# An mLSTM layer with two gated layers on one core: decay products first in each group, the causal mask as a select on GpSimd, loops written out

## The reference

```python
for t in range(S):
    m_new = np.maximum(f_gate[:, :, t] + m, i_gate[:, :, t])
    f_stab = np.exp(f_gate[:, :, t] + m - m_new)
    i_stab = np.exp(i_gate[:, :, t] - m_new)
    m = m_new
    C = f_stab * C + i_stab * np.einsum('bhd,bhe->bhde', vt, kt)
    n = f_stab * n + i_stab * kt
    h_tilde = np.einsum('bhde,bhe->bhd', C, qt)
    denom = np.maximum(np.abs(np.einsum('bhd,bhd->bh', n, qt)), 1.0)
    y[:, :, t] = sigmoid(o_gate[:, :, t]) * h_tilde / denom
x = y as (1536, 320)
xn = x / rms(x) * rms_g
x = (silu(xn @ w_gate) * (xn @ w_val)) @ w_out                 # 320 -> 1536 -> 320
h = x @ w_in; g = max(h, 0) + alpha * min(h, 0)                # 320 -> 2048
out = g @ w_out2                                               # -> 320
```

## Time and profile before

| | |
|---|---|
| median of 3 runs | 508.81 us (507.23 to 510.04) |
| profiled execution | 508.86 us, of which 507.1 us are the span from the first to the last instruction |
| mean granted TensorE clock | 0.996 |
| TensorE busy | 484.6 us (96%) |
| VectorE busy | 319.0 us (63%) |
| GpSimd busy | 233.8 us (46%) |
| ScalarE busy | 212.7 us (42%) |

### The profile page before, as it was taken

How to read it: one execution, slowest core, us unless ns; L and a number is a source line. 1 busy time by engine, 2 the same in 40 slices (tenths; PEclk the granted TensorE clock), 3 DMA queues, 4 the chain that set the end, 5 groups by cost and what they waited for, 6 DMA issues and landing times.

```text
span 507.1 us, 9931 instructions
## 1 busy us (share of the span) xinstructions
PE 484.6 (96%) x3161; PEld 464.2 (92%) x3161; DVE 319.0 (63%) x647; ACT 212.7 (42%) x508; POOL 233.8 (46%) x250
## 2 busy tenths in 40 slices
PE   5998899999999999999999799999999999998996
PEld 4887889998999999998999799999899999997996
DVE  7585896757796484547887366437769622236663
ACT  1442436256535324236545222234654432235652
POOL 3540767536657134244657124331756622225673
PEclk9999999999999999999999899999999999999999
DMA  6778431123434670003435490002243420004562
GB/s 109 165 139 168 129 95 58 51 68 88 114 92 111 121 105 0 1 1 84 124 85 135 90 145 2 1 0 54 88 115 88 89 65 2 1 0 115 137 123 99
DMA packets 80735, 41.31 MB, mean 81 GB/s; under 512 B 51548, under 2 KB 80684, under 8 KB 80684
## 3 DMA queue, kind: packets, MB, share of 16 engines
q1 hardware_dynamic: 80684, 40.65, 35.3%
HBM read 38.67 MB, written 1.97 MB: 80 GB/s over the span
## 4 chain that ended last, share of the span: by engine, by line
PE 75%; DVE 9%; issue 8%; POOL 3%; ACT 2%; DMA 1%; ACTq 0%; DVEq 0%; POOLq 0%; SPq 0%
PE bank L984 36%; PE bank L992 17%; PE bank L995 8%; PE bank L948 2%; PE bank L936 2%; PE bank L912 1%; POOL w L845 1%; DMA shared<-in_moe_w_out 1%; PE bank L889 1%; PE bank L943 1%; POOL hidT L853 1%; PE bank L954 1%; PE bank L926 1%; PE bank L884 1%; PE bank L927 1%
## 5 line engine op out<-in xcount | busy, mean ns | idle before, releaser
L853 POOL TENSOR_TENSOR hidT<-hid,hidT 128x384 fp32r<-128x384 f32 x112 | 118.2, 1055 | 232.3 <-ACT hidT L513 232.0
L513 ACT CAST hidT<-hid 128x384 fp32r<-128x384 f32 x112 | 57.5, 514 | 135.7 <-DVE hid L741 94.1
L984 PE MATMUL bank<-x2T,win 128*128 128x384 f32 x512 | 100.2, 339 | 1.4 <-ACT x2T L554 0.8
L984 PEld LDWEIGHTS bank<-x2T,win 128*128 128x128 f32 x512 | 87.5, 188 | 3.2 <-issue 1.7
L735 DVE SCALAR_TENSOR_TENSOR u<-th,bank 128x384 f32<-128x384 f32 x48 | 26.6, 554 | 92.0 <-ACT th L535 92.0
L984 PE MATMUL bank<-xT,wg 128*128 128x384 f32 x384 | 75.7, 339 | 4.6 <-issue 2.8
L984 PE MATMUL bank<-xT,wv 128*128 128x384 f32 x384 | 77.3, 344 | 0.0
L984 PEld LDWEIGHTS bank<-xT,wg 128*128 128x128 f32 x384 | 66.3, 189 | 6.2 <-issue 5.1
L992 PE MATMUL bank<-w,hidT 128*128 128x320 f32 x384 | 68.4, 313 | 3.5 <-POOL w L845 3.5
L984 PEld LDWEIGHTS bank<-xT,wv 128*128 128x128 f32 x384 | 67.5, 191 | 1.2 <-DVE hid L741 0.3
L758 DVE TENSOR_SCALAR u<-bank,alpha_sb 128x384 f32<-128x384 f32 x64 | 39.4, 616 | 42.3 <-PE bank L984 41.6
(11 more groups left out here) (129 smaller groups left out, 638.2 us busy)
## 6 DMA issues: line engine op xcount, KB each, us to landing
shared<-in_moe_w_out SPq DMA_DIRECT2D x38, 320.0 KB, 5.1
shared<-in_moe_w_in SPq DMA_DIRECT2D x34, 256.0 KB
shared<-in_moe_w_in SPq DMA_DIRECT2D x34, 128.0 KB
q_in<-in_q SPq DMA_DIRECT2D x12, 160.0 KB, 4.4
k_in<-in_k SPq DMA_DIRECT2D x12, 160.0 KB, 4.6
v_in<-in_v SPq DMA_DIRECT2D x12, 160.0 KB, 4.3
o_in<-in_o_gate SPq DMA_DIRECT2D x12, 160.0 KB, 4.4
shared<-in_moe_w_gate SPq DMA_DIRECT2D x6, 256.0 KB
```

Of the source, the lines that this page charges most:

```text
L513: a.copy(hidT[:, i % NH, 0], hid[:, i % 2]).then_inc(s_hid_hi, 1)
L853: gp.tensor_tensor(hidT[:, i % NH, 1], hid[:, i % 2], hidT[:, i % NH, 0].bitcast(F32), ALU.subtract).then_inc(s_hid_lo, 1)
L984: last = te.matmul(dst, w[:, blk, col:col + P], x[:, part, xb, :], start=(n == 0), stop=(n == len(terms) - 1))
```

## The change

These things are changed together.
- In each group D0 and D1 stand ahead of the q and k transposes. So the k transposes now wait for D1's exponential (both use A[2]), D1 waits for `gt_tok` or for C instead (they read A[2]), and `gx` is computed behind D1's exponential. The `norm` of the group before stands between `kT` and S as before, GpSimd's `decay_rhs` for the next group is built at S and `state` instead of D1 and S.
- The mask product is gone. In its place GpSimd zeroes the upper part of `dx` by a select (`causal`), one for each half of the heads, and VectorE's pT waits for it.
- `upd` and `pairmask` are gone; two adds, one for each half of the partitions, take the diagonal blocks from the bank into C.
- The loops over tiles, and SyncE's over weight blocks, are Python loops.
- `maskF` and `maskR` go; the fillers multiply by the identity.

```diff
-    ATT += [("qT", _g), ("kT", _g)] + [("norm", _g - 1)] * (_g > 0) + [("D0", _g), ("D1", _g), ("S", _g)]
+    ATT += [("D0", _g), ("D1", _g), ("qT", _g), ("kT", _g)] + [("norm", _g - 1)] * (_g > 0) + [("S", _g)]
...
-            with eng.Fori(1, NT - 1) as t:
+            for t in range(1, NT - 1):
                 walk(MERGED, mlp, att, weights, t, t + 1)
...
-                with sp.Fori(0, J2 // 4 - 1) as m:
+                for m in range(J2 // 4 - 1):
...
-            with sp.Fori(1, NT - 1) as t:
+            for t in range(1, NT - 1):
...
@@ ScalarE
                     a.copy(kT[0:KP, :, :], quad(A[2])[0:KP]).then_inc(s_kT, 1)
-                    if g == 0:
-                        act.wait_ge(s_gexp_in, t + 1)
-                        act.wait_ge(s_kw, BACK + G * t)
-                        a.activation(gx[:, :, :, :], gexp_in[:, :, :, :], ACT.Exp).then_inc(s_gx, 1)
...
                     a.activation(dx[:, half], quad(A[2 * half]), ACT.Exp).then_inc(s_dx, 1)
+                    if g == 0 and half:
+                        act.wait_ge(s_gexp_in, t + 1)
+                        act.wait_ge(s_kw, BACK + G * t)
+                        a.activation(gx[:, :, :, :], gexp_in[:, :, :, :], ACT.Exp).then_inc(s_gx, 1)
@@ VectorE
-            for r, one in ((0, 0), (REM, 1)):
-                vec.memset(pairmask[r:r + REM, one], 1.0).then_inc(s_const_dve, 1)
-                vec.memset(pairmask[r:r + REM, 1 - one], 0.0).then_inc(s_const_dve, 1)
...
-            vec.tensor_copy(maskR[:, :], maskF[:, :]).then_inc(s_const_dve, 1)
...
                         dve.wait_ge(s_S_mm, BACK + 2 * n + half + 1)
-                        dve.wait_ge(s_dx, 2 * n + half + 1)
+                        dve.wait_ge(s_causal, 2 * n + half + 1)
...
-                    dve.wait_ge(s_upd, n + 1)
+                    dve.wait_ge(s_state_mm, BACK + n + 1)
                     dve.wait_ge(s_C_dec, n + 1)
-                    vec.tensor_tensor(C[0:KP], C[0:KP], upd[0:KP], ALU.add).then_inc(s_C, 1)
+                    for half in range(2):
+                        own = slice(HP * half, HP * half + D)
+                        last = vec.tensor_tensor(C[own, half::2], C[own, half::2], heads(A[2])[own, half::2], ALU.add)
+                    last.then_inc(s_C, 1)
...
-                elif what == "state":
-                    dve.wait_ge(s_state_mm, BACK + n + 1)
-                    dve.wait_ge(s_C, BACK + n)
-                    vec.tensor_tensor(upd[0:KP, :, :].rearrange("p (a b) d -> p a (b d)", b=2), heads(A[2])[0:KP].rearrange("p (a b) d -> p a (b d)", b=2),
-                                      mid(pairmask[0:KP, :, :].rearrange("p b d -> p (b d)"), KP, PAIRS, 2 * DA), ALU.mult).then_inc(s_upd, 1)
@@ GpSimd
-            gp.affine_select(out=maskF[:, :], in_=maskF[:, :], compare_op=ALU.is_ge, fill=-BIG, base=0,
-                             pattern=[[1, P]], channel_multiplier=-1).then_inc(s_const, 1)
...
+            def causal(n, half):
+
+                pool.wait_ge(s_dx, 2 * n + half + 1)
+                gp.affine_select(out=dx[:, half], in_=dx[:, half], compare_op=ALU.is_ge, fill=0.0, base=0,
+                                 pattern=[[0, H // 2], [1, CH]], channel_multiplier=-1).then_inc(s_causal, 1)
...
-                elif what in ("D1", "S") and g < G - 1:
-                    decay(n + 1, g + 1, int(what == "S"))
+                elif what in ("D0", "D1"):
+                    causal(n, int(what[1]))
+                elif what in ("S", "state") and g < G - 1:
+                    decay(n + 1, g + 1, int(what == "state"))
@@ TensorE
-                        pe.wait_ge(s_gate_step, GATE_STEPS * (t + 1)) if g == 0 else pe.wait_ge(s_upd, n)
+                        pe.wait_ge(s_dx, 2 * n + 2)
...
                     if half:
-                        pe.wait_ge(s_kT, n + 1)
+                        pe.wait_ge(s_C, BACK + n) if g else pe.wait_ge(s_gate_step, GATE_STEPS * (t + 1))
...
-                    te.matmul(quad(A[2 * half]), decay_lhs[0:KQ, g * CH:(g + 1) * CH], decay_rhs[0:KQ, half::2, :], start=True, stop=False)
-                    te.matmul(quad(A[2 * half]), identR[:, :], mid(maskR[:, :], P, H // 2, CH), start=False, stop=True).then_inc(s_D_mm, 1)
+                    te.matmul(quad(A[2 * half]), decay_lhs[0:KQ, g * CH:(g + 1) * CH], decay_rhs[0:KQ, half::2, :], start=True, stop=True).then_inc(s_D_mm, 1)
```

More of the change, by code:

```diff
@@ L173, in program @@
         hsum = sb("hsum", [P, H, DA])
-        upd = sb("upd", [P, H, DA])
-        pairmask = sb("pairmask", [P, 2, DA])
         den = sb("den", [P, 3, H])
@@ L202, in program @@
         identR = sb("identR", [P, P], F32R)
-        maskF = sb("maskF", [P, P])
-        maskR = sb("maskR", [P, P], F32R)
         sel = sb("sel", [P, H])
@@ L265, in program @@
         s_dx = sem("s_dx")
+        s_causal = sem("s_causal")
         s_S_mm = sem("s_S_mm")
@@ L272, in program @@
         s_state_mm = sem("s_state_mm")
-        s_upd = sem("s_upd")
         s_C_dec = sem("s_C_dec")
@@ L315, in program @@
         s_group = [sem(f"s_group{g}") for g in range(G)]
-        N_CONST, N_CONST_DVE, GATE_STEPS = 14, 16, 3 * G + 6
+        N_CONST, N_CONST_DVE, GATE_STEPS = 12, 11, 3 * G + 6
         BACK = 3
@@ L800, in _ @@
                 pool.sem_inc(held, BACK)
-            for ap, value in ((ident[:, :], 0.0), (maskF[:, :], 0.0), (sel[:, :], 0.0), (minus_half[:, :], -0.5),
+            for ap, value in ((ident[:, :], 0.0), (sel[:, :], 0.0), (minus_half[:, :], -0.5),
                               (q_in[:, :, :, D:HP], 0.0), (k_in[:, :, :, D:HP], 0.0), (kw[:, :, D:HP], 0.0), (v_in[:, :, :, D:DA], 1.0)):
                 gp.memset(ap, value).then_inc(s_const, 1)
-            pool.wait_ge(s_const, 8)
+            pool.wait_ge(s_const, 7)
             gp.affine_select(out=ident[:, :], in_=ident[:, :], compare_op=ALU.not_equal, fill=1.0, base=0,
                              pattern=[[-1, P]], channel_multiplier=1).then_inc(s_const, 1)
-            gp.affine_select(out=maskF[:, :], in_=maskF[:, :], compare_op=ALU.is_ge, fill=-BIG, base=0,
-                             pattern=[[1, P]], channel_multiplier=-1).then_inc(s_const, 1)
             for r in range(4):
-                pool.wait_ge(s_const, 10 + r)
+                pool.wait_ge(s_const, 8 + r)
                 gp.affine_select(out=sel[:, :], in_=sel[:, :], compare_op=ALU.not_equal, fill=1.0, base=-32 * r,
@@ L883, in _ @@
             for _ in range(WARM_UP):
-                te.matmul(quad(GV[1]), identR[:, :], mid(maskR[:, :], P, 4, CH), start=True, stop=True)
+                te.matmul(quad(GV[1]), identR[:, :], mid(identR[:, :], P, 4, CH), start=True, stop=True)
             def keep(count):
                 for _ in range(count):
-                    te.matmul(quad(GV[1]), identR[:, :], mid(maskR[:, :], P, 4, CH), start=True, stop=True)
+                    te.matmul(quad(GV[1]), identR[:, :], mid(identR[:, :], P, 4, CH), start=True, stop=True)
             def att(what, g, t):
@@ L964, in att @@
                     elif g == 1:
-                        pe.wait_ge(s_upd, G * t + G)
+                        pe.wait_ge(s_C, BACK + G * t + G)
                     else:
```

## The result

The kernel became slower: 515.49 us, median of 4 runs (515.1 to 515.68), against 508.68 us for the kernel before on the same chip (4 runs, 507.23 to 510.04). The ratio is 1.0135, 95% interval 1.0108 to 1.0161. The forecast was 508.1, slightly faster, with a range of 503.8 to 512.0; the kernel is 6.8 us slower and lies above that range. The profiled execution took 515.31 us with a span of 513.5, that is 6.4 us of span more than before.

The account below looks back on a forecast made before the run. TensorE, busy 96% of the span, was taken to bound the kernel. From 508.86 us: -2.8 and +0.6 (mask product), -4.5 (loops), +2.8 (opening), +2.9 (first tile), +0.2 (looped tiles) gave 508.1, range 503.8 to 512.0.

Parts of the forecast that it names:

- step 3: Opening, 11 to 46 us: D0 and D1 first lengthen the serial chain; +2.8 us, bounds +1 and +4.
- Rival G: Opening: the clock falls there too, as TensorE idles 1.3 and 0.6 us; +1.7 us, 509.8; chance 0.06.
- Step 2: Loops written out: the stall at the jump back and the slow clock behind it go; together -4.5 us.
- Rival F: Jump between tiles: the stop at 284 us stays in straight code; 4.5 us more, 512.6; chance 0.08.
- Step 1: Mask product removed on TensorE: -2.8 us in the two looped tiles, +0.6 given back at the `out2` 0 wait.
- step 5: Looped tiles: D0 stalls 0.1 us each for its right-hand side, other new waits are covered; +0.2 us.
- Step 4: First tile: D0 waits 4.2 us for GpSimd's `decay_rhs` and the clock falls behind it; +2.9 us.
- rival C: First tile: TensorE waits, but the clock stays up; 1.7 us less, 506.4; chance 0.13.
- B: First tile: TensorE does not wait, as GpSimd reaches the decays earlier; 4.3 us less, 503.8; chance 0.11.
- D: Opening costs only 0.5 us, as fillers give way and exponentials overlap the transposes; 505.8; chance 0.12.
- rival E: GpSimd's select costs much more than its rows scale to, deciding from about 1.2 us on; +5 us, 513; chance 0.08.

## Why the prediction was wrong

**What failed is step 3, the opening**: +8.8 where it had +2.8, outside its own bounds of +1 and +4. Two things in it were off, and only the second is large.

The chain itself, at full clock, came to +4.2 instead of +2.8 (the kernel with fillers). Group 0 was right: S +1.6 at 17.14, the walk said 17.1. From there to S of group 1 it grew by 0.85 (walk 0.6), from `hsum` to S of group 2 by 1.7 (walk 1.5). The rest is in the parts on VectorE. The walk took 0.9 off between S of group 1 and its `hsum`, because `upd` goes; measured is -0.3. There the scaling of C, 0.92 before, takes 1.32. It now begins near the start of a weight split on GpSimd, where before it began near its end, and so most of the saved 0.49 is given back. Between S of group 2 and its `hsum` it grew by 0.4 where the walk had nothing.

The clock cost 4.6 us. The step put D0 at 13.4 and wrote "Before, the transposes of q and k lay in the time of that wait", and didn't ask what TensorE does in that time once they are gone: it idles for 2.47 us, and again for 0.68 and 1.49 before the later groups. Rival G named the effect, but at 1.3 and 0.6 us of idleness, one fall of the clock and 1.7 us, with a chance of 0.06. The prediction itself had, for the first tile, the premise that an idle stretch brings the clock down; it was not applied to the one place of the kernel where TensorE has the least to do. The opening is a serial chain with nothing to hide a slow stretch behind, and here there were several in a row.

**Step 2, the loops, was right**: -4.5 forecast, -4.4 measured with this edit alone. Rival F is out.

**Step 1, the mask products, was right in size and nearly in sum.** In the old order a tile gains 1.40, so the 0.2 a tile that I set against `out2` 0 did not show there; with D0 first 0.38 a tile comes back, against 0.3 forecast (0.2 in step 1, 0.1 in step 5).

**Step 5 failed at "Other new waits are covered"**: 0.84 a tile in three tiles, by the decay product that moved to `state`. I checked the queue of each engine for what stands behind what, but not what runs beside what. The kernel with both decays at S shows it: that one step moved takes the wait away.

**Step 4, the first tile: the sum hit (+2.6 against +2.9, and 0.2 from step 1), the wait was right, and the clock term was wrong.** D0 starts 4.06 us later than the q transposes stood, forecast 4.2. Only 2.33 of it is idleness, because TensorE's clock fell behind the stall of 1.78 us for `u` and it came to D0 late; but GpSimd's right-hand side sets D0's start, so this low clock cost nothing more. Behind the wait for D0, where I had put 1.7 for the clock, it stayed full, as rival C had it. Two terms that I didn't have took its place: 0.59 for the low clock that the opening left behind in the first `gate` projections, and 0.84 for the x2 transposes. With what goes (six masks 1.4, the waits of 0.6 for `gt_tok` and 0.5 for the exponential) this gives 4.06 + 0.59 + 0.84 - 2.5 = +3.0, against 2.63 measured; some 0.3 is not accounted for. That the sum agreed is luck: 1.7 that did not come stood for 1.4 that were left out. Taking D0's wait away gave back 1.94 and no more, since the low clock behind the stall then counts. B (no wait) and D (a cheap opening) are out.

**The select.** 0.61 forecast, 0.64 measured without other work beside it (median; the mean in the changed kernel is 0.72): rival E is out. The sentence "At either it is hidden" was wrong as a general claim. In the old order the opening is 2 us longer with the select. It queues behind `norm`, and pT waits 1.3 us for it; moving `norm` gave back 0.57. Doubling it makes the opening up to 2 us longer again, part of that by the clock. In the changed order `norm` stands behind the selects, and no wait for pT stands in the list of TensorE's waits. The two adds to C were put at 0.32 each and took 0.323.

What stays open: why the 1.78 us stall in the first tile brings the clock down in some kernels and not in others (below). In the changed kernel it costs nothing, as it lies in the wait for D0; in the three kernels without that wait (weight pieces behind the gates, and the two with repairs) D0 starts 9.36 or 9.37 us behind the stall, against 7.81 for the step at that place before. Some 0.3 us of the first tile stay open too.

## What to carry to other kernels

An order that puts a step first puts it ahead of its input as well: for each such step look up what the engine did in the time of the wait, and in a serial stretch put work or fillers there, or the clock is lost on top of the wait (here 4.6 us on 4.2). But ask of a slow stretch what it delays: where the next step waits for another engine anyway, it costs nothing. When a step moves, look at what it will run beside, not only at what is queued behind it: VectorE and GpSimd products in the same stretch took 1.3 to 2.7 times as long as with nothing beside them. And take bundled changes apart: here loops, select and state gained 5.0 us in the old order (503.3 against 508.3), and the reordering that came with them cost 12.2 (515.5 against 503.3).

## What the runs showed of the hardware that was not expected

- The clock does not follow the length of a single stall. Every one of these kernels has the same wait of 1.78 us for `u` in the first tile. From 1 us before its end to 7 us behind, the granted clock was 0.79 in nine of them (the changed kernel, its four single repairs, the two with repairs together, all but the order, each select twice) and 1.00 in five (the kernel before, only the loops, loops and select, all but the order with more fillers, the same with `norm` moved). Before the last `xT` transposes of the opening, 2.34 and 2.35 us of idleness left the clock at 1.00 (old order in the opening only, repairs together), while 2.34 and 2.33 us were followed by 0.50 for at least 2 us (loops and select, 48 to 50 us; all but the order, 46 to 48 us).
- A product on GpSimd beside VectorE's slows both: 1.04 to 1.36 us on GpSimd, 1.31 to 2.16 for two splits on VectorE. The scaling of C takes 0.49 with nothing beside it and 1.32 in group 1 of the changed opening, beside a weight split.
- GpSimd's select is close to linear in its columns (0.19, 0.29 and 0.64 us for 8, 128 and 512) and cheaper than a two-operand product of the same size (1.04).
- At the jump back of the loop TensorE stopped for 2.79 us, with nothing that the profile shows to wait for; no instruction of ScalarE, VectorE or GpSimd began between 284.21 and TensorE's next at 286.88. The slow clock behind it cost 1.6 (4.4 saved without the jump, less 2.79) to 1.8 us (7.38 - 5.61).
